# Halves of O added by an fp32 product on TensorE, normalised from PSUM; 1e-9 added on GpSimd

## What is computed

```python
q_rot, k_rot = (rotate(q), rotate(k))
scale = 1.0 / np.sqrt(D)
scores = scale * np.matmul(q_rot, k_rot.transpose(0, 1, 3, 2))
scores = scores - np.max(scores, axis=-1, keepdims=True)
attn = np.exp(scores)
attn = attn / (np.sum(attn, axis=-1, keepdims=True) + 1e-09)
return np.matmul(attn, v).astype(np.float32)
...
xt = x.transpose(0, 2, 1)
h = np.maximum(xt @ w_tok1, 0.0) @ w_tok2
u = x + h.transpose(0, 2, 1)
h2 = np.maximum(u @ w_ch1, 0.0) @ w_ch2
return (u + h2).astype(np.float32)
```

## Time and profile before

| | us |
|---|---|
| median of 3 runs | 747.25 |
| lowest and highest | 746.81 and 749.2 |
| the profiled execution | 748.91 |
| its span | 747.1 |
| TensorE busy | 702.6 (94%) |
| VectorE busy | 420.4 (56%) |
| ScalarE busy | 347.0 (46%) |
| GpSimd busy | 224.0 (30%) |

### The profile page before, as it was taken

The page is one execution under the profiler, slowest core; times in us unless marked ns, Lnnn a source line. Parts: engine busy times, 40 slices in busy tenths (PEclk is TensorE's granted clock), DMA queues, the critical chain, the costliest instruction groups (busy, mean ns, idle before and its releaser), DMA issues.

```text
span 747.1 us, 13082 instructions
## 1 busy us (share of the span) xinstructions
PE 702.6 (94%) x5104; PEld 658.5 (88%) x5104; DVE 420.4 (56%) x676; ACT 347.0 (46%) x743; POOL 224.0 (30%) x224
## 2 busy tenths in 40 slices
PE   2799999999999999988899999999999999999996
PEld 1698888888888888887699998999989999899996
DVE  6689999999999999887652213212232122221211
ACT  3578888888888888876440203202122021220110
POOL 2977776676777766221000000000000000000000
PEclk9999999999999999999999999999999999999999
DMA  8656665565555555770520001200002000010000
GB/s 226 148 125 158 158 157 141 147 153 145 143 138 146 134 148 124 187 253 17 185 72 1 29 1 36 71 2 29 1 35 70 0 28 0 0 37 1 29 1 35
DMA packets 58422, 65.57 MB, mean 88 GB/s; under 512 B 18432, under 2 KB 42112, under 8 KB 58368
## 3 DMA queue, kind: packets, MB, share of 16 engines
q1 hardware_dynamic: 58368, 64.84, 32.5%
HBM read 29.16 MB, written 9.44 MB: 52 GB/s over the span
## 4 chain that ended last, share of the span: by engine, by line
PE 49%; DVE 1%; ACT 1%; issue 0%; ACTq 0%
PE slot L899 14%; PE slot L898 14%; PE slot L897 14%; PE slot L938 4%; PE slot L931 1%; PE slot L985 1%; PE slot L166 1%; PE slot L169 1%; ACT x_hi L149 1%; PE slot L168 0%; DVE x_lo L154 0%; DVE x_hi L158 0%; ACTq L862 0%; DVE out_t L1109 0%; DVE out_t L1106 0%
## 5 line engine op out<-in xcount | busy, mean ns | idle before, releaser
L615 ACT ACTIVATE prob<-slot,neg_max 128x576 f32<-128x576 f32 x160 | 117.8, 737 | 47.5 <-DVE neg_max L705 47.5
L705 DVE TENSOR_REDUCE neg_max<-slot 128x1 f32<-128x576 f32 x160 | 118.5, 752 | 20.4 <-PE slot L491 19.4
L1031 ACT ACTIVATE h_hi<-slot 128x512 fp32r<-128x512 f32 (+1 forms) x48 | 31.3, 651 | 184.3 <-PE slot L899 184.3
L897 PE MATMUL slot<-ut_hi,w_ch_hi 128*128 128x320 f32 (+1 forms) x384 | 114.0, 297 | 0.0
L899 PE MATMUL slot<-ut_hi,w_ch_lo 128*128 128x320 f32 (+1 forms) x384 | 113.7, 296 | 0.0
L898 PE MATMUL slot<-ut_lo,w_ch_hi 128*128 128x320 f32 (+1 forms) x384 | 113.7, 296 | 0.0
L897 PE MATMUL slot<-h_hi,w_ch_hi 128*128 128x320 f32 (+1 forms) x384 | 113.7, 296 | 0.0
L898 PE MATMUL slot<-h_lo,w_ch_hi 128*128 128x320 f32 (+1 forms) x384 | 113.7, 296 | 0.0
L899 PE MATMUL slot<-h_hi,w_ch_lo 128*128 128x320 f32 (+1 forms) x384 | 113.7, 296 | 0.0
L1076 DVE SCALAR_TENSOR_TENSOR h_lo<-slot,h_hi 128x512 fp32r<-128x512 f32 (+1 forms) x56 | 41.5, 748 | 119.6 <-ACT h_hi L1031 112.9
L488 PE MATMUL slot<-key,q_hi 128*128 128x288 f32 x320 | 83.4, 343 | 9.0 <-DMA key<-t_lo_k 5.1
(11 more groups left out here) (87 smaller groups left out, 1323.4 us busy)
## 6 DMA issues: line engine op xcount, KB each, us to landing
q_hi<-t_hi_q SPq DMA_DIRECT2D x32, 160.0 KB, 2.4
q_cross<-t_lo_q SPq DMA_DIRECT2D x32, 160.0 KB, 2.6
q_cross<-t_hi_q SPq DMA_DIRECT2D x32, 160.0 KB, 2.8
key<-t_hi_k SPq DMA_DIRECT2D x32, 160.0 KB, 2.6
key<-t_lo_k SPq DMA_DIRECT2D x32, 160.0 KB, 3.0
raw_qk<-in_q_dram SPq DMA_DIRECT2D x16, 256.0 KB, 2.9
raw_qk<-in_k_dram SPq DMA_DIRECT2D x16, 256.0 KB, 3.0
raw_v<-in_v_dram SPq DMA_DIRECT2D x16, 256.0 KB, 3.3
```

The source lines that it names most:

```text
L615: act.activation(prob[a][:, t, 0:S].rearrange("p (f n) -> p f n", f=2), slot[(a * NG + t) % 2][:, :, 0:HALF], ACT.Exp, bias=neg_max[a][:, ...
L705: dve.tensor_reduce(neg_max[a][:, t:t + 1], slot[(a * NG + t) % 2][:, :, 0:HALF], AX.XY, ALU.max, negate=True).then_inc(maxed[t], 1)
L897: pe.matmul(ps, lhs[0], rhs[0], start=first, stop=False)
L1031: act.activation(h2[0][:, 2 * i:2 * i + 2, 0:n], unit_slot(k)[:, :, 0:n], ACT.Relu).then_inc(hi_done, 1)
```

## The change

The addition of 1e-9 moves from VectorE (`tail_and_sum`) to GpSimd (`guard`, at the head of its step). GpSimd makes a 128x64 matrix `both`, the sum of the two halves of the identity: two identities above each other. `transpose_o` multiplies `ot` by `both` as an ordinary fp32 product, five times with 64 moving columns; so the halves are added on the way, and O takes 320 columns of one bank. `output` on VectorE multiplies these from PSUM by the inverse sums and writes the pair's block. `normalise` and `o_sum` are gone. `x_pair` becomes two blocks with a semaphore each. `invert` moves to just before `output`, a step later than before.

```diff
...
@@ -195,10 +195,11 @@
     N = B * H
     UNROLL = 4
     UNIT_BANK = (3, 0, 1, 2, 3, 2)
-    T_SLOT, V_SLOT, O_SLOT = slot[2], slot[3], slot[2]
+    T_SLOT, V_SLOT = slot[2], slot[3]
+    O_BANK = slot[2][:, 1, :]
 
     raw = {"q": raw_qk[:, 0], "k": raw_qk[:, 1]}
-    x_pair = sb(ctx, "x_pair", [P, NG, 2, D])
+    x_pair = [sb(ctx, f"x_pair{a}", [P, NG, 2, D]) for a in range(2)]
     raw["v"] = sb(ctx, "raw_v", [P, 2, NG, D])
     by_cos = sb(ctx, "by_cos", [P, 2, NG, D])
     by_sin = sb(ctx, "by_sin", [P, 2, NG, D])
@@ -219,9 +220,10 @@
     total = [sb(ctx, f"total{a}", [P, NG]) for a in range(2)]
     guarded = [sb(ctx, f"guarded{a}", [P, NG]) for a in range(2)]
     inverse = [sb(ctx, f"inverse{i}", [P, NG]) for i in range(UNROLL)]
-    o_sum = [sb(ctx, f"o_sum{a}", [P, NG, D]) for a in range(2)]
     stage = [stage_or_x[:, n * CH:(n + 1) * CH] for n in range(2)]
     zeros = sb(ctx, "zeros", [P, NG, D])
+    both = sb(ctx, "both", [P, D])
+    eps = sb(ctx, "eps", [P, NG])
 
     rope_in = {n: sem(f"rope_in_{n}") for n in "qk"}
     raw_in = {n: sem(f"raw_in_{n}") for n in "qkv"}
...
@@ -323,9 +325,9 @@
             def store(p):
 
                 sp.dma_start(x_scratch[p][0:MAIN, :].rearrange("(p t) c -> p t c", t=G),
-                             x_pair[:, 0:G].rearrange("p t h d -> p t (h d)")).then_inc(x_stored, 16)
+                             x_pair[p % 2][:, 0:G].rearrange("p t h d -> p t (h d)")).then_inc(x_stored[p % 2], 16)
                 sp.dma_start(x_scratch[p][MAIN:S, :],
-                             x_pair[0:TAIL, G].rearrange("p h d -> p (h d)")).then_inc(x_stored, 16)
+                             x_pair[p % 2][0:TAIL, G].rearrange("p h d -> p (h d)")).then_inc(x_stored[p % 2], 16)
 
             for i, n in enumerate("qk"):
                 tables = slice(i * 2 * NG * D, (i + 1) * 2 * NG * D)
...
@@ -404,9 +407,12 @@
             pool.memset(ident[:], 0.0).then_inc(consts, 1)
             pool.memset(zeros[:], 0.0).then_inc(consts, 1)
             pool.memset(ot[:, S:W], 0.0).then_inc(consts, 1)
-            pool.wait_ge(consts, 3)
+            pool.memset(eps[:], 1e-9).then_inc(consts, 1)
+            pool.wait_ge(consts, 4)
             pool.affine_select(out=ident[:], in_=ident[:], compare_op=ALU.not_equal, fill=1.0, base=0,
                                pattern=[[-1, P]], channel_multiplier=1).then_inc(consts, 1)
+            pool.wait_ge(consts, 5)
+            pool.tensor_tensor(both[:], ident[:, 0:D], ident[:, D:P], ALU.add).then_inc(consts, 1)
 
             def split_v(a, h):
 
@@ -421,24 +427,21 @@
                 pool.tensor_tensor(v_sb[a][:, :, D:P], raw["v"][:, a], f32(v_sb[a][:, :, 0:D]),
                                    ALU.subtract).then_inc(v_split, 1)
 
-            def normalise(i, h):
-
-                if no(h):
-                    return
-                a = i % 2
-                pool.wait_ge(o_summed, h + 1)
-                pool.wait_ge(inv_done, h + 1)
-                if a == 0 and not early(h):
-                    pool.wait_ge(x_stored, h * 16)
-                pool.tensor_tensor(x_pair[:, :, a, :], o_sum[a][:],
-                                   inverse[i][:].unsqueeze(2).broadcast_to([P, NG, D]), ALU.mult).then_inc(x_done, 1)
+            def guard(h):
+
+                if no(h):
+                    return
+                pool.wait_ge(exped[NG - 1], h + 1)
+                if h >= 2:
+                    pool.wait_ge(inv_done, h - 1)
+                pool.tensor_tensor(guarded[h % 2][:], total[h % 2][:], eps[:], ALU.add).then_inc(guard_done, 1)
 
             for m in (2, 3):
                 rotate(pool, "qk"[m % 2], m)
 
             def step(i, s, rotation=True):
+                guard(s - 1)
                 split_v((i - 1) % 2, s - 1)
-                normalise((i - 3) % UNROLL, s - 3)
                 if rotation:
                     rotate(pool, "qk"[i % 2], s + 4)
 
...
@@ -517,8 +520,10 @@
                 if not (isinstance(h, int) and h + 2 >= N - 2):
                     pe.wait_ge(t_lo_done, h + 5)
                 pe.wait_ge(ot_done, h + 1)
+                if early(h):
+                    pe.wait_ge(consts, 6)
                 for t in range(NG):
-                    mm = pe.transpose(flat(O_SLOT)[:, t * P:(t + 1) * P], ot[:, t * P:(t + 1) * P], ident[:])
+                    mm = pe.matmul(O_BANK[:, t * D:(t + 1) * D], ot[:, t * P:(t + 1) * P], both[:], start=True, stop=True)
                 mm.then_inc(o_ready, 1)
 
             def turn_p(a, h, u):
@@ -536,7 +541,7 @@
                     pass
                 elif u < 3:
                     if not early(h):
-                        pe.wait_ge(o_summed, h)
+                        pe.wait_ge(x_done, h)
                     elif u == 1:
                         pe.wait_ge(t_lo_done, 4)
                 else:
@@ -612,6 +617,8 @@
                 if no(h):
                     return
                 act.wait_ge(maxed[t], h + 1)
+                if t == 0 and h >= 2:
+                    act.wait_ge(guard_done, h - 1)
                 act.activation(prob[a][:, t, 0:S].rearrange("p (f n) -> p f n", f=2),
                                slot[(a * NG + t) % 2][:, :, 0:HALF], ACT.Exp,
                                bias=neg_max[a][:, t:t + 1], accum_out=total[a][:, t:t + 1]).then_inc(exped[t], 1)
@@ -723,14 +730,6 @@
                     dve.tensor_tensor(pt_lo[:, :, MAIN:S], ps[:, 0:G * TAIL].rearrange("p (j n) -> p j n", j=G),
                                       f32(pt_hi[:, 0:G, MAIN:S]), ALU.subtract).then_inc(pt_lo_done[u], 1)
 
-            def tail_and_sum(i, h):
-
-                if no(h):
-                    return
-                a = i % 2
-                dve.wait_ge(exped[NG - 1], h + 1)
-                dve.tensor_scalar(guarded[a][:], total[a][:], 1e-9, None, ALU.add).then_inc(guard_done, 1)
-
             def invert(i, h):
 
                 if no(h):
@@ -743,10 +742,11 @@
                 if no(h):
                     return
                 dve.wait_ge(o_ready, h + 1)
-                if not early(h - 1):
-                    dve.wait_ge(x_done, h - 1)
-                dve.tensor_reduce(o_sum[a][:], flat(O_SLOT)[:, 0:W].rearrange("p (t i d) -> p t d i", t=NG, i=2), AX.X,
-                                  ALU.add).then_inc(o_summed, 1)
+                dve.wait_ge(inv_done, h + 1)
+                if a == 0 and h >= 4:
+                    dve.wait_ge(x_stored[h // 2 % 2], h // 4 * 32)
+                dve.tensor_tensor(x_pair[h // 2 % 2][:, :, a, :], O_BANK[:, 0:NG * D].rearrange("p (t d) -> p t d", t=NG),
+                                  inverse[h % UNROLL][:].unsqueeze(2).broadcast_to([P, NG, D]), ALU.mult).then_inc(x_done, 1)
 
             def weights_lo(c):
                 dve.wait_ge(w_hi_done, c + 1)
@@ -767,13 +767,12 @@
             def step(i, s, turn=True):
                 a = i % 2
                 maximum(a, s, 0)
-                tail_and_sum((i - 1) % UNROLL, s - 1)
                 maximum(a, s, 1)
-                invert((i - 1) % UNROLL, s - 1)
                 if turn:
                     t_part_lo("qk"[a], (i // 2 + 1) % 2, s + 2)
                 maximum(a, s, 2)
                 maximum(a, s, 3)
+                invert((i - 2) % UNROLL, s - 2)
                 output(a, s - 2)
                 p_lo(s - 1, 0)
                 p_lo(s - 1, 5)
...
```

More of the change, by code:

```diff
@@ L85, in build @@
         w1 = ChannelWeights(nc, whole, w_ch1_whole, wc1)
-        x_stored = whole.enter_context(nc.semaphore("x_stored"))
+        x_stored = [whole.enter_context(nc.semaphore(f"x_stored{n}")) for n in range(2)]
         token = TokenProducts(nc, whole, stage_or_x, x_hi, x_lo, wt1, x_scratch)
@@ L239, in attention @@
     pv_ready, ot_done = sem("pv_ready"), sem("ot_done")
-    o_ready, o_summed, x_done = sem("o_ready"), sem("o_summed"), sem("x_done")
+    o_ready, x_done = sem("o_ready"), sem("x_done")
     guard_done, inv_done = sem("guard_done"), sem("inv_done")
@@ L359, in step @@
                     if isinstance(s, int) and s == N - UNROLL:
-                        sp.wait_ge(x_stored, 32 * (s // 2 - 2))
+                        for n in range(2):
+                            sp.wait_ge(x_stored[n], 16 * (s // 2 - 2))
                         sp.wait_ge(w_lo_done, len(chunks))
@@ L449, in _ @@
                     step(i, quad * UNROLL + i)
-            for s in range(N - UNROLL, N + 3):
+            for s in range(N - UNROLL, N + 1):
                 step(s % UNROLL, s, rotation=False)
@@ L458, in transpose_qk @@
                 if early(m):
-                    pe.wait_ge(consts, 4)
+                    pe.wait_ge(consts, 5)
                 elif early(m - 1):
@@ L790, in _ @@
                 step(s % UNROLL, s, turn=s < N - 2)
-            tail_and_sum(3, N - 1)
-            invert(3, N - 1)
             dve.wait_ge(products, 2 * N)
@@ L795, in _ @@
             token.split_lo(dve, 0, 1)
+            invert(2, N - 2)
             output(0, N - 2)
```

(4 more changed lines are left out.)

## The result

| | before | after |
|---|---|---|
| median of four runs each, us | 747.11 (746.81 to 749.2) | 757.24 (756.1 to 758.04) |
| ratio, with its 95% interval | 1 | 1.0128 [1.0104, 1.0153] |
| the profiled execution, us | 748.91 | 756.1 |
| its span, us | 747.1 | 754.2 |

The change makes the kernel slower by 10.1 us, 1.3%. The forecast was 758.7 us, inside 741.5 to 777.5, with slower at 0.65.

What follows compares the result with a forecast made beforehand. The prediction took a loop of waits between TensorE, ScalarE and VectorE to bound the kernel. Its terms, -4.9 - 1 + 17.2 + 0.2 = +11.5 us, gave 760.4 against the profiled run, 758.7 as a median; range 741.5 to 777.5.

Steps and rivals of the forecast that it cites:

- The O products: On TensorE ahead of the turned P: five fp32 products at 0.22 us replace transposes at 0.109, +17.2 us.
- Rival 1: TensorE's fp32 products as cheap as the transposes, 0.107 to 0.13 us each: 741.4 to 743.9 us; chance 0.25.
- Rival 3: On TensorE nothing is hidden, or four loads, over 0.28 us a product: 777.4 or 792 us; chance 0.2.
- The addition: Moving the 1e-9 from VectorE to GpSimd shortens the loop by 0.21 us in 22 steps, plus 0.3: -4.9 us.
- the two kinds of step: Attention loop steps of 10.06 us where VectorE's addition takes 0.76 us, and 9.84 where it takes 0.18.
- Rival 4: GpSimd's new addition collides with the reciprocal, or its head-of-step wait makes the rotation late: 763.6 us; chance 0.05.
- VectorE's output: Multiplication and reciprocal of about 0.65 us replace 0.81; only 0.03 us of slack a step counts: -1 us.
- the first hand-over: From TensorE's first turned unit of P to ScalarE's copy, with hardly 0.06 us of slack.
- its round: The loop of waits through TensorE, ScalarE's copy of P and VectorE's pt_lo: 5.78 + 0.68 + 3.38 = 9.84 us.
- Rival 5: VectorE's saving counts whole, 30 x 0.16 us more: 737.5 us with cheap products; chance 0.02.
- the 10.35 named as a sign: Successors of TensorE's L468 transpose were to start about 10.35 us apart in every step.
- Tail: After the last O product: +0.55 for the products, about -0.35 for the shorter output, +0.2 us.

Runs made afterwards that it cites:

- experiment 2: The changed kernel with the addition of 1e-9 back on VectorE in its old place: 763.78 us, ratio 1.0219.
- experiment 1: The kernel before with only the 1e-9 addition moved to GpSimd and the reciprocal moved a step later; transposes and reduction stay: 741.9 us, ratio 0.9925.
- experiment 3: The changed kernel with 64 instead of 128 weight columns in each O product, half of the output not computed: 749.88 us, ratio 1.0041.
- experiment 4: The changed kernel with 32 instead of 64 moving columns in each O product, half of O's columns not computed: 758.42 us, ratio 1.014.
- experiment 5: The changed kernel with `ot` and `both` as fp32r, one weight load a product, low part of O lost: 739.78 us, ratio 0.9902.
- experiment 8: The changed kernel with the O transposes back and VectorE's multiplication reading only the high half: 740.01 us, ratio 0.9897.
- experiment 6: The kernel before without the 1e-9 addition, the reciprocal taken of the plain sums in its old place: 741.77 us, ratio 0.9917.
- experiment 7: The kernel before with the addition still on VectorE, but as a sum of two SBUF tensors: 747.49 us, ratio 0.9993.

## Why the prediction was right

**The O products, +17.2 forecast, +16.4 measured** (experiment 2, with the output and the tail in it). Like for like the forecast was 17.2 - 1 + 0.2 = 16.4 as well; the changed kernel against experiment 1 gives 15.3. The price of 0.22 us a product was an estimate, and it came out at 0.223 us (ten loads 0.111 apart), the block longer by 0.53 us instead of 0.555. Experiments 3 and 4 show that weight columns set it and that moving columns, at 64 and fewer, do not; experiment 5 shows that one load instead of two takes all of it away. Rival 1, products as cheap as transposes, fell: the block was to be 0.55 to 0.65 us and was 1.08. Rival 3, nothing hidden or four loads, fell too: the half products are hidden, and there are two loads. Of the two pages of the Trainium skill that the prediction weighs, "TensorE: Matmul & The Clock Gate", Terms, with its 4 times for the transpose mode, gave 0.218 us. The trace's 0.223 is near it, but by chance: an estimate by the same rule halves the price for 32 columns, and experiment 4 measured it unchanged. "FP8 and Floating Point Precision", TensorE Precision Notes, with its four passes, gave 0.107, and the measurement decides against it as a price.

**The addition, -4.9 forecast, -5.5 measured** (experiment 1; 0.16 us on the mean of the loop's steps, 10.03 to 9.87, so 4.2 over 26 of them). Reading the two kinds of step in the trace, and not 32 x 0.75 us, was the right sum. But a step without the addition is 9.87 us and not 9.84, so a long step gives back 0.18 and not 0.21, and that the total still came to 5.5 is luck: the other 1.3 us lie outside these steps, and no run shows where. GpSimd's cover held. Rival 4 fell: no wait of TensorE for the rotation between 40 and 340 us, the reciprocal at 180 ns.

**VectorE's output, -1 forecast, about 0 measured.** This is the term that was off in relation to its size. The 0.03 us between ScalarE's end and pt_lo's start was counted as slack that a faster VectorE would close. Experiments 1 and 8 have the same 0.03 to 0.04 us with the reduction and without: it is the hand-over from ScalarE. ScalarE's copy sets this start, and what VectorE saves ahead of it becomes waiting. The 0.06 us at the first hand-over weren't slack either: ScalarE's copy starts 0.03 us after TensorE's unit ends where it waits for it (158.61 and 158.64 in the changed kernel), and in the kernel before it had just come from the exp of the third score tile. The prediction left this second way, from the score tile by VectorE's maximum and the exp, out of its round. It cost the forecast nothing, because the O products only lengthen the other one. Rival 5 (0.16 us a step back) falls with it. This term and the 9.87 us are why the steps are 10.40 us and not the 10.35 named as a sign.

**Tail, +0.2 forecast, +0.17 seen** from the start of the last O products to that of the last token products (2.35 to 2.52 us). The rest of the hand-over was shorter, with TensorE waiting for its sequencer (PEq) 0.87 instead of 1.28 us; nothing was run to say why.

Sum: -5.5 + 16.4 = +10.9 by parts, +10.1 measured together, +11.5 forecast. That the parts come to 0.8 more is inside their intervals (about 0.002 each, 1.5 us), and one reason for a difference shows in the steps: the addition costs 0.23 us beside the O products and 0.16 without them. What stays open is where the 1.3 us of the addition's gain outside the steps lie, and what the granted clock at the hand-over adds or takes.

## What to carry to other kernels

Price a true fp32 product with few moving columns (64 here; more were not run) by its weight loads, two for each, and look at what stands behind it: five products on the round trip of a loop cost five times 0.11 us more than five transposes in each step, and halving what they move saved nothing. A saving on VectorE counts only in the stretch where VectorE arrives last: of the 23 us of its work that went, about 5.5 came back, all of it from the addition. And a tiny VectorE addition with its operands in SBUF is not tiny beside a busy GpSimd: giving it to the engine that has time (experiment 1), or dropping it where it changes nothing (experiment 6), was worth 5.5 and 6.2 us (the second by its ratio), and both are versions that beat the kernel before and the changed one, 741.9 and 741.8 us.

## What the runs showed of the hardware that was not expected

- A true fp32 product appears as two weight loads and two matmuls. Their pace is 0.111 us a load for 128 weight columns, 0.058 for 64, and the same for 64 and for 32 moving columns.
- Of the 0.53 us by which experiment 3's loads are shorter, 0.27 is lost at the two ends of the block, where TensorE goes from 128 to 64 weight columns and back. That the switch is the cause is not shown.
- The 0.75 us of a five-column addition is the rest of GpSimd's running instruction, in the scalar and in the two-tensor form alike (80 of 80); the reciprocal of five columns takes 0.17 to 0.19 us in the same kernels and in experiments 1 and 6, beside a running GpSimd too (154.26 us in the kernel before, where GpSimd's instruction ran from 153.61 to 154.48).
- Near its start the program runs its score products at 0.85 us a pair, and 0.54 later, and the five transposes of q or k take 1.27 us instead of 0.74, with the granted clock given as 1.00 in both stretches. The changeover came at about 31 us in the changed kernel's profile, between 31 and 33 in experiment 7's and after 37 in that of before:

```profile
36.27 0.85 PE L488 MATMUL slot<-key,q_hi 128*128 128x288 f32 x2
```

```profile
31.42 0.54 PE L491 MATMUL slot<-key,q_hi 128*128 128x288 f32 x2 [0.56 <-ACT prob L622]
```

Why it differs from one execution to the next was not tried.
